# The q/k products of a fused attention and gated-MLP kernel: a loop on TensorE over four buffers of 3, 3, 3 and 2 tiles, late tiles in buffers of their own, and squares summed three tiles at a time

## The reference, cut to what matters

```python
# attention over the channels; q, k, v are [1, 6016, 256] in float32
qn = q / (norm(q, axis=1) + 1e-6)          # column norms: sums of squares over all 6016 rows
kn = k / (norm(k, axis=1) + 1e-6)
s = kn.transpose(0, 2, 1) @ qn / tau       # 256 x 256
a = softmax(s, axis=-1)
x = v @ a                                  # 6016 x 256
# then two gated layers, 256 -> 1536 -> 256 each
xn = x / sqrt(mean(x*x) + 1e-6) * rms_g
x = (silu(xn @ w_gate) * (xn @ w_val)) @ w_out
out = (sigmoid(x @ w2_gate) * (x @ w2_val)) @ w2_out
```

## Time and profile before

| | |
|---|---|
| median of 3 runs | 1245.74 us (1245.04 to 1246.05) |
| profiled execution | 1245.01 us |
| span of its trace | 1243.2 us |
| TensorE busy | 1235.9 us, 99% |
| VectorE busy | 684.3 us, 55% |
| ScalarE busy | 457.1 us, 37% |
| share of TensorE in the chain that ended last | 97% |

### The profile page before, as it was taken

How to read it: one execution, slowest core, us unless ns; L and a number is a source line. 1 busy time by engine, 2 the same in 40 slices (tenths; PEclk the granted TensorE clock), 3 DMA queues, 4 the chain that set the end, 5 groups by cost and what they waited for, 6 DMA issues and landing times.

```text
span 1243.2 us, 15544 instructions
## 1 busy us (share of the span) xinstructions
PE 1235.9 (99%) x5572; PEld 1038.0 (83%) x5572; DVE 684.3 (55%) x1141; ACT 457.1 (37%) x744; POOL 31.0 (2%) x25
## 2 busy tenths in 40 slices
PE   9999999999999999999999999999999999999998
PEld 8788888888888888888888888888888888889888
DVE  7887655554555554555555455555455555545343
ACT  6654433333333333333333333333333333333332
POOL 0003500000000000000000000000000000000000
PEclk9999999999999999999999999999999999999999
DMA  9930000100100100100010010010010000000000
GB/s 371 278 104 1 1 7 3 35 0 9 34 0 9 34 0 9 34 0 9 6 28 0 9 34 0 9 34 0 9 34 0 9 14 16 1 7 17 1 17 13
DMA packets 63186, 37.01 MB, mean 30 GB/s; under 512 B 51384, under 2 KB 54840, under 8 KB 63160
## 3 DMA queue, kind: packets, MB, share of 16 engines
q1 hardware_dynamic: 61928, 35.81, 10.0%
q10 hardware_dynamic: 1232, 0.85, 0.2%
HBM read 30.48 MB, written 6.18 MB: 29 GB/s over the span
## 4 chain that ended last, share of the span: by engine, by line
PE 97%; ACT 1%; DMA 1%; DVE 1%; SPq 0%; issue 0%; DVEq 0%
PE ps L867 21%; PE ps L869 21%; PE ps L868 21%; PE ps L1039 10%; PE ps L1041 10%; PE ps L1040 10%; PE ps L965 2%; DMA tau_c<-in_tau 0%; DMA qk<-in_k 0%; SPq L272 0%; PE ps L931 0%; DVE xs_lo L742 0%; ACT L456 0%; PE ps L884 0%; DVE x_lo L575 0%; DVE out_sb L569 0%
## 5 line engine op out<-in xcount | busy, mean ns | idle before, releaser
L800 DVE TENSOR_TENSOR h<-ps,h 128x512 f32<-128x512 f32 (+1 forms) x276 | 187.7, 680 | 249.1 <-PE ps L869 236.5
L494 ACT ACTIVATE h_hi<-h 128x512 fp32r<-128x512 f32 (+1 forms) x276 | 171.6, 622 | 362.8 <-DVE h L800 362.8
L489 ACT ACTIVATE h<-ps 128x512 f32<-128x512 f32 (+1 forms) x276 | 162.2, 588 | 329.4 <-PE ps L869 317.8
L805 DVE TENSOR_TENSOR h_lo<-h,h_hi 128x512 fp32r<-128x512 f32 (+1 forms) x276 | 187.9, 681 | 139.0 <-ACT h_hi L494 137.2
L1041 PE MATMUL ps<-h_hi,w_lo_o 128*128 128x512 f32 (+1 forms) x576 | 221.5, 385 | 0.0
L1039 PE MATMUL ps<-h_hi,w_hi_o 128*128 128x512 f32 (+1 forms) x576 | 221.5, 385 | 0.0
L1040 PE MATMUL ps<-h_lo,w_hi_o 128*128 128x512 f32 (+1 forms) x576 | 221.5, 385 | 0.0
L796 DVE TENSOR_TENSOR h<-ps,h 128x512 f32<-128x512 f32 (+1 forms) x132 | 89.7, 679 | 138.5 <-ACT h L489 138.5
L1041 PEld LDWEIGHTS ps<-h_hi,w_lo_o 128*128 128x128 f32 x576 | 108.1, 188 | 20.6
L1039 PEld LDWEIGHTS ps<-h_hi,w_hi_o 128*128 128x128 f32 x576 | 108.1, 188 | 20.6
L1040 PEld LDWEIGHTS ps<-h_lo,w_hi_o 128*128 128x128 f32 x576 | 108.1, 188 | 20.5
(11 more groups left out here) (142 smaller groups left out, 1337.5 us busy)
## 6 DMA issues: line engine op xcount, KB each, us to landing
v_in<-in_v SPq DMA_DIRECT2D x44, 128.0 KB, 3.0
out<-out_sb SPq DMA_DIRECT2D x44, 128.0 KB, 2.4
qk<-in_q SPq DMA_DIRECT2D x7, 512.0 KB, 8.6
qk<-in_k SPq DMA_DIRECT2D x7, 512.0 KB, 9.5
w_raw_g<-in_moe_w_gate SPq DMA_DIRECT2D x6, 512.0 KB, 8.5
w_raw_v<-in_moe_w_val SPq DMA_DIRECT2D x6, 512.0 KB, 9.7
w_raw_o<-in_moe_w_out SPq DMA_DIRECT2D x6, 512.0 KB, 10.6
qk<-in_q SPq DMA_DIRECT2D x9, 256.0 KB, 5.1
```

The lines of the kernel that those rows point to most:

```text
L489: nc.scalar.activation(h[:, slot, 0:w], ps[:, GATE[slot], 0:w], ACT.Sigmoid).then_inc(sig_done, 1)
L494: nc.scalar.activation(h_hi[:, part, 0:w], h[:, slot, 0:w], ACT.Copy).then_inc(hi_done, 1)
L800: nc.vector.tensor_tensor(h[:, slot, 0:w], ps[:, VALUE[slot], 0:w], h[:, slot, 0:w], ALU.mult).then_inc(h_done, 1)
L805: nc.vector.tensor_tensor(h_lo[:, part, 0:w], h[:, slot, 0:w], h_hi[:, part, 0:w].bitcast(F32), ALU.subtract).then_inc(lo_done, 1)
```

## The change

The 47 tiles are cut anew. Three early chunks of 1, 2 and 2 tiles have a buffer each. Twelve chunks go three times round four buffers of 3, 3, 3 and 2 tiles. Four late chunks of 3, 2, 2 and 2 tiles have a buffer each, so that their loads wait for no buffer. A load in the second and third turn waits for the chunk four before it. On TensorE the three turns are a hardware loop, whose waits compare with a register's value. VectorE adds a whole chunk with one instruction, up to three tiles wide. After the first late chunk it folds the third tile's width into the first, and after the last one the second into the first. `column_norms` comes after six late c = 0 products in place of five. The wait for `tau` and its reciprocal come behind the inverse norms, and the spread waits for these alone. The second `vt_low` comes behind the first score, and `first_x` waits for the halves of v one by one. The two products of `warm_up` have 512 and 128 columns, from one broadcast column, and their constant is written first.

```diff
-QK_TILES = 4
-QK_SLOTS = 6
-LATE = 4
-NORMS_BEHIND = 5
+EARLY = (1, 2, 2)
+ROUND = (3, 3, 3, 2)
+ROUNDS = 3
+LATE = (3, 2, 2, 2)
+NORMS_BEHIND = 6
...
-    sizes = [1] + [2] * 5 + [QK_TILES] * ((TILES - 19) // QK_TILES) + [2] * LATE
+    sizes = EARLY + ROUND * ROUNDS + LATE
...
             for i, slot, t0, n in chunks:
-                if i >= QK_SLOTS:
-                    sp.wait_ge(qk_multiplied, i - QK_SLOTS + 1)
-                    sp.wait_ge(qk_squared, i - QK_SLOTS + 1)
+                if turn_of(i):
+                    sp.wait_ge(qk_multiplied, i - len(ROUND) + 1)
+                    sp.wait_ge(qk_squared, i - len(ROUND) + 1)
...
+            nc.gpsimd.memset(ones[:, :], 1.0).then_inc(const_ready, 1)
             nc.gpsimd.memset(ident[:, :], 0.0).then_inc(const_zero, 1)
-            nc.gpsimd.memset(ones[:, :], 1.0).then_inc(const_ready, 1)
...
                 dve.wait_ge(qk_squared, i + 1)
-                for lo in range(0, n * C, 2 * C):
-                    hi = min(lo + 2 * C, n * C)
-                    dve.wait_ge(qk_summed, sums_through(i - 1) + lo // (2 * C))
-                    nc.vector.tensor_tensor(sum_sq[:, :, 0:hi - lo], sum_sq[:, :, 0:hi - lo],
-                                            sq_qk[:, i % 2, :, lo:hi], ALU.add).then_inc(qk_summed, 1)
+                dve.wait_ge(qk_summed, sums_through(i - 1))
+                nc.vector.tensor_tensor(sum_sq[:, :, 0:n * C], sum_sq[:, :, 0:n * C],
+                                        sq_qk[:, i % 2, :, 0:n * C], ALU.add).then_inc(qk_summed, 1)
+                if i == CHUNKS - len(LATE):
+
+                    dve.wait_ge(qk_summed, sums_through(i))
+                    nc.vector.tensor_tensor(sum_sq[:, :, 0:C], sum_sq[:, :, 0:C], sum_sq[:, :, 2 * C:3 * C], ALU.add)\
+                      .then_inc(sums_folded, 1)
+                    dve.wait_ge(sums_folded, 1)
...
-            dve.wait_ge(tau_loaded, 16)
-            nc.vector.reciprocal(inv_tau, tau_c[:, :]).then_inc(soft_step, 1)
             vt_low(0, 0, x2)
-            vt_low(0, 1, x2)
             dve.wait_ge(norm_ready, 1)
             nc.vector.tensor_scalar(norm_e, norm, 1e-6, None, ALU.add).then_inc(soft_step, 1)
-            dve.wait_ge(soft_step, 2)
+            dve.wait_ge(soft_step, 1)
             nc.vector.reciprocal(inv, norm_e).then_inc(soft_step, 1)
+            dve.wait_ge(tau_loaded, 16)
+            nc.vector.reciprocal(inv_tau, tau_c[:, :]).then_inc(soft_step, 1)
...
             score(0)
+            vt_low(0, 1, x2)
...
-                pe.wait_ge(vt_lo_done, CC)
                 for c in range(CC):
+                    pe.wait_ge(vt_lo_done, c + 1)
...
-            warm_up(5)
-            for i, slot, t0, n in chunks[:-LATE]:
-                pe.wait_ge(qk_loaded[slot], 32 * (i // QK_SLOTS + 1))
-                for t in range(n):
-                    for c in range(CC):
-                        mm = raw(slot, t, c, t0 + t)
-                mm.then_inc(qk_multiplied, 1)
+            warm_up(4 * P, P)
+            for i, slot, t0, n in chunks[:len(EARLY)]:
+                pe.wait_ge(qk_loaded[slot], 32)
+                raw_chunk(slot, n, first=(i == 0))
+            with pe.Fori(0, ROUNDS) as turn:
+                for slot, n in enumerate(ROUND, len(EARLY)):
+                    pe.wait_ge(qk_loaded[slot], turn * 32 + 32)
+                    raw_chunk(slot, n)
...
-            pe.wait_ge(soft_step, 3)
+            pe.wait_ge(soft_step, 2)
```

More of the change, by code:

```diff
@@ L55, in build, with slot_of, turn_of @@
     assert CC == 2 and N % P == 0 and 0 < TAIL and FULL >= 4 and J % 6 == 0
-    sizes = [1] + [2] * 5 + [QK_TILES] * ((TILES - 19) // QK_TILES) + [2] * LATE
+    sizes = EARLY + ROUND * ROUNDS + LATE
     assert sum(sizes) == TILES
-    chunks = [(i, i % QK_SLOTS, sum(sizes[:i]), n) for i, n in enumerate(sizes)]
-    CHUNKS = len(chunks)
+    CHUNKS, WIDEST = len(sizes), max(sizes)
+    homes = EARLY + ROUND + LATE
+    HOME = [sum(homes[:i]) for i in range(len(homes))]
+    def slot_of(i):
+        if i < len(EARLY):
+            return i
+        if i < len(EARLY) + len(ROUND) * ROUNDS:
+            return len(EARLY) + (i - len(EARLY)) % len(ROUND)
+        return i - len(ROUND) * (ROUNDS - 1)
+    def turn_of(i):
+        return (i - len(EARLY)) // len(ROUND) if slot_of(i) in range(len(EARLY), len(EARLY) + len(ROUND)) else 0
+    chunks = [(i, slot_of(i), sum(sizes[:i]), n) for i, n in enumerate(sizes)]
+    LATE_CHUNKS = chunks[-len(LATE):]
     def sums_through(i):
-        return 1 + sum(-(-n // 2) for n in sizes[:i + 1])
+        return 2 + i
     def narrow(b):
@@ L183, in build @@
         o2_copied = sem("o2_copied")
-        qk_loaded = [sem(f"qk_loaded{i}") for i in range(QK_SLOTS)]
+        qk_loaded = [sem(f"qk_loaded{i}") for i in range(len(homes))]
         qk_multiplied, qk_squared, qk_summed = sem("qk_multiplied"), sem("qk_squared"), sem("qk_summed")
@@ L955, in column_norms, with warm_up @@
                 mm.then_inc(norms_made, 1)
-            def warm_up(n):
+            def warm_up(*widths):
                 pe.wait_ge(const_ready, 1)
[L960 to L967, removed]
@@ L970, in _, with raw @@
-            warm_up(5)
-            for i, slot, t0, n in chunks[:-LATE]:
-                pe.wait_ge(qk_loaded[slot], 32 * (i // QK_SLOTS + 1))
+                for n in widths:
+                    nc.tensor.matmul(ps[:, Y[1], 0:n], ones[:, :], ones[:, 0:1].broadcast_to([P, n]),
+                                     start=True, stop=True)
+            def raw(slot, n, t, c, first=False, last=False):
+                part = at_home(slot, n)
+                return nc.tensor.matmul(ps[:, RAW[c], 0:C], alternate(part[:, 1, t * C:(t + 1) * C], c),
+                                        part[:, 0, t * C:(t + 1) * C], start=first, stop=last)
@@ L973, in _, with raw_chunk @@
+            def raw_chunk(slot, n, first=False):
                 for t in range(n):
                     for c in range(CC):
-                        mm = raw(slot, t, c, t0 + t)
+                        mm = raw(slot, n, t, c, first=(first and t == 0))
                 mm.then_inc(qk_multiplied, 1)
+            warm_up(4 * P, P)
[6 more added lines that the diff above has]
+                    raw_chunk(slot, n)
@@ L977, in late_raw @@
             def late_raw(c, first, end):
-                for i, slot, t0, n in chunks[-LATE:]:
+                for i, slot, t0, n in LATE_CHUNKS:
                     for tile in range(max(first, t0), min(end, t0 + n)):
                         if c == 0 and tile == t0:
-                            pe.wait_ge(qk_loaded[slot], 32 * (i // QK_SLOTS + 1))
-                        mm = raw(slot, tile - t0, c, tile)
+                            pe.wait_ge(qk_loaded[slot], 32)
+                        mm = raw(slot, n, tile - t0, c, last=(tile == TILES - 1))
@@ L984, in late_raw @@
                 return mm
-            late = chunks[-LATE][2]
+            late = LATE_CHUNKS[0][2]
             pe.wait_ge(const_ready, 4)
```

24 lines of the change are left out of this document (13 added, 11 removed).

## The result

Each kernel ran five times, alternating on one chip. The changed kernel took 1252.63 us in the median (1251.78 to 1252.77), the kernel before 1245.74 us (1245.04 to 1246.05): a ratio of 1.0053, with an interval of 1.0042 to 1.0063. It is slower by 6.9 us, where 1247.7 us had been forecast, with 1249.8 as the upper end of the range. The profiled execution took 1251.78 us, 6.8 us more than that of before.

A forecast was written before the change was run, and what follows sets the result against it. TensorE's own work bounds the kernel; the opening stage's products and VectorE's fold end together. Later norms +2.17, +0.43 and -0.64 make +1.96 us on 1245.01: 1247.0, or 1247.7 us as median; range 1245.1 to 1249.8 us.

The forecast's parts named there:

- chunk 13's issue: SyncE's queue in the opening stage: issued when chunk 9 is multiplied, after 25 tiles, at 26.50 us.
- The time of a load: Ring loads: a three-tile chunk lands 4.1 us after issue, 2.19 us fixed plus 1.92 us at 410 GB/s.
- the late chunks don't bind: End of the opening stage: the last load lands at about 37.6 us, before VectorE comes to it at 40.4 us.
- The clock stays at 1.00: TensorE behind the 2.6 us pause before the norms: granted clock stays at 2.4 GHz, adding nothing to the sum.
- The fall: Rival: clock drops to 1.2 GHz in the new pause before the norms, +2 us, about 1249.7 us; chance 0.15.
- The `tau` wait: Between norms and spread: VectorE's wait for `tau` leaves the path whole, -0.64 us (bounds -0.36 and -0.75).
- One product more behind the norms: TensorE after the norms: 12 products left where 11 were, +0.43 us.
- TensorE's arrival: Before the norms: 82 products instead of 83, so TensorE arrives at 39.9 us, then waits 2.6 us for the fold.
- The loop: TensorE's hardware loop in the opening stage: its turns cost 0.
- two signs of being wrong: Profile after: prediction is wrong if the fold ends before 41 us or TensorE pauses at a turn of the loop.
- A single late engine: Rival: a DMA load comes 1.25 us late on chunk 13, moving the fold as much, 1248.9 us; chance 0.12.
- The fold is in time after all: Rival: loads keep ahead, TensorE doesn't wait at the norms, only the `tau` gain remains, 1245.1 us; chance 0.12.

The follow-up runs named there:

- e3: The changed kernel with four extra products of 512 columns, their result overwritten, ahead of the norms: 1249.43 us, ratio 1.0029.
- e1: The kernel before with only the `tau` wait and reciprocal behind the inverse norms, and the second half's split behind the first score: 1245.73 us, ratio 1.0000.
- e12: The changed kernel with chunk 2's k load moved from ScalarE's queue to SyncE's, ahead of chunk 3's loads: 1251.87 us, ratio 1.0048.
- e4: The changed kernel with three-tile chunks round six buffers (18 tiles), loop written out, late chunks in the ring, both folds last: 1246.95 us, ratio 1.0010.
- e8: The changed kernel with two extra products of 512 columns, their result overwritten, ahead of the norms: 1250.13 us, ratio 1.0036.
- e2: The changed kernel with TensorE's hardware loop written out: 1251.77 us, ratio 1.0048.
- e7: The changed kernel with every three-tile add split into one of two tiles and one of one: 1252.52 us, ratio 1.0052.
- e9: The same kernel as e4 with five buffers of three tiles in the ring (15 tiles) instead of six: 1248.54 us, ratio 1.0017.
- e6: The changed kernel with the norms behind 14 late products in place of 6, and the spread behind all products: 1250.58 us, ratio 1.0040.
- e5: The kernel before with only the loads of chunks 6 to 12 waiting for the chunk three before, not six: 1254.69 us, ratio 1.0066.

## Why the prediction was wrong

The chain was the right one: reach, chunk 13's issue, sums, fold, norms. Two of its steps failed. Of the miss of 4.9 us, e3 puts 3.2 on the clock and leaves 1.7 for the late fold; in the traces the two are nearer, 2.4 and 2.2 us.

**The time of a load, and with it "the late chunks don't bind"**, is the first. The forecast had VectorE without a gap from 32.1 us on, and the fold ending at 42.5; it ended at 44.66. Of the 2.17 us:

- 1.10 us lie ahead of chunk 13's square. It was issued at 27.27 us and not at 26.50, because TensorE had waited for chunk 2 until 7.97 us instead of 7.20. In part that is chance: e1, with the opening loads of the kernel before, had chunk 2 at 7.64 us. Then chunk 13 took 4.43 us to land and not 4.1 (0.33).
- 1.07 us are VectorE's wait for chunk 15. Chunks 14 and 15 (five tiles, 1.31 MB) landed in 4.28 us after chunk 13, where 410 GB/s, taken from the earlier trace rows, gives 3.2. The engines moved 358 GB/s in these 4.28 us, 1.53 MB, so some of it belonged to loads issued behind chunk 15.

The other traces say which part is the rule. Chunk 13 was issued at 26.82 us in e3 and at 26.66 in e12, close to the forecast's 26.50, and the fold still ended at 44.43 and 44.28 us. Over the seven traces with the changed kernel's ring, chunk 13's square began 4.5 to 5.6 us after its issue, where 4.1 had been forecast; the changed kernel's own 4.47 us is the shortest. So it is the time that a load takes in this ring that was mis-sized, more than its issue. The forecast itself had named rates near 300 GB/s for the ring, and they came (305), but it sized the loads at 410. That rate is one of a queue that is full for many microseconds. Here 305 GB/s stand beside a share of 0.91: the engines were held most of the time and moved less in it. e4, with nearly the same load sizes and a longer queue, moved 400 GB/s at 1.03; so it isn't the size of a load.

The Trainium skill's 0.6 us to the first byte ("DMA: Bandwidth & Descriptors", "Latency and other measured facts") would have put the fold at 40.9 us, further off still. The trace goes the other way: even the 2.19 us taken in its place were too little here.

**"The clock stays at 1.00", the forecast's term of nothing**, is the second. The fall was a rival, held at 0.15 and priced at 2 us. It happened, and cost 3.2 us by e3. The weighing failed by its argument "it is short beside the stage". A pause of 2.6 us without a fall did happen in e8, so the chance wasn't senseless; but the pause came out at 3.66 us through the first failure, and the two were taken as independent. The Trainium skill's rule that idle time brings the clock down ("TensorE: Matmul & The Clock Gate", Part 1) was the warning, and the trace agrees with its direction: 0.50 from 45 to 50 us. The ten passes behind the norms took 3.93 us against 2.04: twice, as the rival said.

**The `tau` wait** (-0.64) is right in kind and smaller: -0.43 in e1, -0.46 in e3 (3.31 us against 3.77). "So this wait goes whole" is wrong at full clock: TensorE's weight loads waited 0.27 us in e1 and 0.35 in e3 before the spread, because GpSimd's root took 1.32 and 1.41 us where 1.02 was counted on. In the changed kernel the slow clock hid that: norms and products take longer than VectorE's part, so +1.85 stands in its place, and that TensorE didn't wait before the spread, as forecast, was luck. **One product more behind the norms** (+0.43): +0.43 in e3 (47.80 to 51.58, 3.78 us against 3.35), +0.54 with the low clock. The norms' position cost nothing else that shows: e4 has it, and its trace is 0.6 us from the one before.

**Right:** TensorE's arrival (39.9 forecast; its passes end at 40.66 us, which is 39.9 and the 0.77 of chunk 2). The warm-up: chunk 1 begins at 5.29 us as before. Squares and adds of three tiles, from the groups by shape to 44.6 us:

```profile
L606 DVE TENSOR_TENSOR sum_sq<-sum_sq,sq_qk 128x1536 f32<-128x1536 f32 x10 | 17.6, 1758 | 7.4 <-ACT sq_qk L410 7.2
L410 ACT ACTIVATE sq_qk<-qk 128x1536 f32<-128x1536 f32 x10 | 14.8, 1485 | 9.2 <-DMA qk<-in_k 9.2
```

1.76 and 1.48 us, as worked out. The loop: 0, as taken (e2). The adds' number: 0 (e7). That everything from the opening stage stays in the time was right too: 6.73 of 6.77 us.

**Slips in its working.** Chunk 13 holds tiles 34 to 36, not 31 to 33, and the load that came late in the earlier trace rows had been issued twelve microseconds before, not ten; nothing in the sum rests on either. Neither of its two signs of being wrong (a fold before 41 us, a pause at a turn) came, although it was wrong: both looked for a fold that is too early or for the loop, none for a fold that is too late.

**The rivals that fell.** A single late engine (0.12) isn't what came: the rate was low over the whole ring. "The fold is in time after all" fell with the late issue of chunk 13, which came even later than forecast.

**What stays open.** What makes the clock fall. Pauses of TensorE of 2.62 us (e8) kept it, 1.62 (e9) and 2.76 (e6) didn't; 3.66 in the changed kernel, 4.44 in e7 and 4.62 in e5 gave 6.8 us at the low level, 3.67 in e2 and 3.90 in e12 gave 3.4. It fell inside the pause in the changed kernel and 1.5 us behind the pause's end in e2. The length of the pause alone doesn't decide. Nor do the runs tell why the engines move less in the same share while the queue runs short, or why chunk 2 comes late.

## What to carry to other kernels

A ring's length is counted in the time of a load under the traffic that the ring itself makes, not in that of an unhurried load and not at the rate of a full queue. In this kernel a shorter ring made both worse at once, the issue and the rate. A buffer of its own doesn't make a load early when it is issued in order behind one that waits. And where a forecast puts a new pause before work on TensorE, add the lower clock behind it to the price, and don't call a pause safe because it is short: here 1.62 us was followed by the fall, and 2.62 us wasn't.

## What the runs showed of the hardware

- The granted clock fell after a pause as short as 1.62 us (e9) and stayed through one of 2.62 us (e8); what it cost in the changed kernel was 3.2 us by the medians of e3.
- A DMA share of 0.91 with 305 GB/s stands beside 1.03 with 400 GB/s (e4), for loads of nearly one size: the share doesn't say how much is moved.
- TensorE began with chunk 2 at 7.52 to 7.97 us with its k load on ScalarE's queue (the changed kernel and five variants) and at 7.06 us with it on SyncE's (e12). That it gains time is not shown.
- A hardware loop round 22 products a turn showed no gap on TensorE: 152 passes in 32.69 us, 0.215 each, as without it.
